# Narrow unread products in TensorE's waits of the first routing round, and four wide ones ahead of its list in place of eight

## The reference

```python
logits = x @ w_gate
flat = logits.flatten()
order = np.argsort(-flat)
for idx in order:
    tok, e = (int(idx) // E, int(idx) % E)
    if assigned[tok] >= 0 or counts[e] >= cap:
        continue
    assigned[tok] = e
    counts[e] += 1
out = np.zeros((N, D), dtype=np.float32)
for e in range(E):
    mask = assigned == e
    h = np.maximum(x[mask] @ w1[e], 0.0)
    out[mask] = h @ w2[e]
```

## Time and profile before

| what | us |
|---|---|
| median of 3 runs | 1098.61 |
| lowest, highest | 1098.16, 1103.46 |
| the profiled execution | 1097.65 |
| its span in the trace | 1095.7 |
| TensorE busy in it | 1056.4 |
| VectorE busy in it | 597.8 |

### The profile page before, as it was taken

The page is one execution under the profiler, slowest core; times in us unless marked ns, Lnnn a source line. Parts: engine busy times, 40 slices in busy tenths (PEclk is TensorE's granted clock), DMA queues, the critical chain, the costliest instruction groups (busy, mean ns, idle before and its releaser), DMA issues. The chain is left out here.

```text
span 1095.7 us, 20355 instructions
## 1 busy us (share of the span) xinstructions
PE 1056.4 (96%) x7565; PEld 903.8 (82%) x7565; DVE 597.8 (55%) x2189; ACT 460.5 (42%) x1172; POOL 422.7 (39%) x472
## 2 busy tenths in 40 slices
PE   9899999999999999999999999948999998999998
PEld 7688888888888888888888888837777786779987
DVE  6754747464747475656556554365675755653110
ACT  5765444444444444444444432203333333234442
POOL 1363222222222222222222224206476647567873
PEclk9999999999999999999999999959999999999999
DMA  6663112121212121212120000014334343324420
GB/s 192 211 206 134 56 56 74 54 70 40 70 55 74 55 73 35 71 55 74 49 70 30 30 11 20 1 38 165 127 143 153 135 156 106 135 97 151 176 106 29
DMA packets 23251, 98.20 MB, mean 90 GB/s; under 512 B 3008, under 2 KB 5056, under 8 KB 20960
## 3 DMA queue, kind: packets, MB, share of 16 engines
q0 software_dynamic: 9824, 58.99, 15.2%
q1 hardware_dynamic: 13328, 37.90, 10.6%
HBM read 84.30 MB, written 12.85 MB: 89 GB/s over the span
## 5 line engine op out<-in xcount | busy, mean ns | idle before, releaser
L427 POOL TENSOR_TENSOR g_low<-g,g_high 128x256 fp32r<-128x256 f32 x192 | 155.1, 808 | 470.8 <-ACT g_high L646 470.7
L536 PE MATMUL up_ps<-x_high,w_high 128*128 128x256 f32 x768 | 227.7, 296 | 0.0
L536 PE MATMUL up_ps<-x_low,w_high 128*128 128x256 f32 x768 | 216.1, 281 | 0.0
L536 PE MATMUL up_ps<-x_high,w_low 128*128 128x256 f32 x768 | 215.1, 280 | 0.0
L814 DVE SCALAR_TENSOR_TENSOR g<-g,up_ps 128x256 f32<-128x256 f32 x192 | 80.4, 419 | 237.0 <-ACT g L639 237.0
L646 ACT ACTIVATE g_high<-g 128x256 fp32r<-128x256 f32 x192 | 80.3, 418 | 209.7 <-PE down_ps L549 140.6
L536 PEld LDWEIGHTS up_ps<-x_high,w_high 128*128 128x128 f32 x768 | 144.5, 188 | 10.7 <-issue 7.7
L549 PE MATMUL down_ps<-w_high,g_high 128*128 128x512 f32 x384 | 152.1, 396 | 0.5 <-POOL g_low L427 0.5
L549 PE MATMUL down_ps<-w_high,g_low 128*128 128x512 f32 x384 | 151.4, 394 | 0.0
L549 PE MATMUL down_ps<-w_low,g_high 128*128 128x512 f32 x384 | 151.2, 394 | 0.0
L536 PEld LDWEIGHTS up_ps<-x_low,w_high 128*128 128x128 f32 x768 | 144.8, 189 | 2.7
(11 more groups left out here) (222 smaller groups left out, 1836.5 us busy)
## 6 DMA issues: line engine op xcount, KB each, us to landing
qk_t<-qk_rows SPq DMA_DIRECT2D x20, 720.0 KB, 4.3
v_w<-v_win SPq DMA_DIRECT2D x40, 232.0 KB
w_raw<-weights SPq DMA_DIRECT2D x16, 512.0 KB, 5.7
x_rest<-x_any POOLq DMA_DIRECT2D x24, 256.0 KB, 3.1
x_rows<-x POOLq DMA_DIRECT2D x12, 512.0 KB, 3.2
w_raw<-gate_rows SPq DMA_DIRECT2D x1, 2048.0 KB, 7.2
qk_t<-qk_rows SPq DMA_DIRECT2D x3, 512.0 KB, 4.4
v_w<-v_win SPq DMA_DIRECT2D x8, 128.0 KB
```

Source lines behind the costliest of these rows:

```text
L427: pool.tensor_tensor(g_low[:, u % 2, :], g[:, u % 2, :], g_high[:, u % 2, :].bitcast(F32), ALU.subtract)\
L536: last = nc.tensor.matmul(up_ps[:, u % 2, 0:GT * P], a[:, f, w], x[:, grp % 2, c, :], start=k == 0, stop=k == 3 * C - 1)
```

## The change

`keep_busy` takes a number of columns, by default 96, half of what it had. The loop over the parts of round 0 is written out, and unread products are put between its parts: 11 narrow ones ahead of the first count, one between a count and its digit, four between a digit and the next count (two after the last digit), three behind the count of the wins, two between the list and its spread. Ahead of the list stand four of 192 columns in place of eight. The 17 behind the spread stay.

```diff
-            def keep_busy(count):
+            def keep_busy(count, columns=T * E // 2):
 
 
                 for _ in range(count):
-                    nc.tensor.matmul(down_ps[:, CT - 1, 0:T * E], ident[:, :], logits[:, :], start=True, stop=True)
-
-            for k in range(SPREAD + 1):
-                route(0, k)
-                if k == SUMS:
-                    keep_busy(8)
-                if k == SPREAD:
-                    keep_busy(17)
+                    nc.tensor.matmul(down_ps[:, CT - 1, 0:columns], ident[:, :], logits[:, 0:columns], start=True, stop=True)
+
+            keep_busy(11)
+            for lv in range(NL):
+                count(0, lv)
+                keep_busy(1)
+                digit(0, lv)
+                keep_busy(4 if lv < NL - 1 else 2)
+            count_wins(0)
+            keep_busy(3)
+            sum_marks(0)
+            keep_busy(4, T * E)
+            list_tokens(0)
+            keep_busy(2)
+            spread_tokens(0)
+            keep_busy(17, T * E)
             for p in range(E):
                 products(p)
```

## The result

The changed kernel is slower by half a percent: 1105.51 us as the median of 20 runs (1102.28 to 1113.76), against 1102.11 us for the kernel before, timed beside it in 20 runs (1097.26 to 1107.52). The ratio is 1.0046, with a 95% interval from 1.0025 to 1.0067: about 5 us more, 3 to 7 by the interval. The profiled execution of the changed kernel is one of the long ones, 1113.73 us with a span of 1111.9, so its end says little. The first routing round is read from it.

The account below looks back on a forecast made before the run. The first routing round was taken as bound by a serial TensorE-VectorE chain at the lower clock, and before the list by the filler itself. Terms -1.6 + 0.4 + 0.5 - 0.4 + 0.1 = -1.0 us; forecast 1097.7, range 1095.3 to 1101.5.

Parts of the forecast that it names:

- The list: Ahead of the token list in round 0: four wide products in place of eight, -1.6 us whatever the clock does.
- The price of a filler: A narrow fp32 pass, taken as bound by its weight load: 0.11 us at the upper clock, 0.21 at the lower.
- The entry: 11 fillers ahead of the first count: nothing at the upper clock, +1.2 at the lower; taken as +0.4 us.
- The levels: Fillers between counts and digits: hidden at the upper clock, 0.5 us each at the lower; one of six assumed, +0.5 us.
- lower level throughout: Rival, also the low rival: lower clock for the whole first routing round, +3.7 us, so 1102.3 us; chance 0.12.
- Marks and spread: Wins' products and counts faster, -0.4 us together; two fillers behind the list delay the spread, +0.1 (+0.6 at the lower clock).
- What it passes on: Behind the tokens' indices: the summed -1.0 us moves gathers and second weights as one; the 17 wide fillers stay hidden.
- The rule on idle gaps: Skill's rule blaming clock drops on long idle gaps; by it the clock-holds rival is expected, 1097.2 us, chance 0.23.
- The later stretches at the lower clock: Rival: a clock fall from 907.6 on, costing 1.6 us, vanishes or another appears: 1096.1 or 1099.3 us; chance 0.08.

Follow-up runs that it names:

- no_entry: The changed kernel without the 11 fillers at the entry; one run, 1104.30 us.
- narrow_48: The changed kernel with narrow fillers of 48 columns in place of 96; one run, 1106.24 us.
- list_as_before: The changed kernel with eight wide fillers ahead of the list again and none behind it; one run, 1105.90 us.

## Why the prediction was wrong

**The list** was right in the step and in the price. -1.6 us from eight fillers to four: the list's start moved by 1.61 us relative to the marks' sums, and the tokens are read 4.18 us behind them (742.80 to 746.98), where the prediction had 4.1. Alone it brought 1.3 at the indices, since with four the clock is still low at the list and its spread.

**The price of a filler** was right for a pass: 0.21 us at the lower level was forecast, (4.98 - 0.4) / 21 = 0.22 measured, and the two runs with 48 columns and with bf16 leave the fp32 weight load as what sets it. By the time that the Trainium skill ("TensorE: Matmul & The Clock Gate", section "LDWEIGHTS (loading the stationary operand)") gives for a load, passes would have been bound by streaming, 0.16 us at the lower level; they are 0.22.

**The entry** is where the prediction failed first. "If it rises after some 3 us here" was taken from eight wide fillers and carried to narrow ones. In the profiled execution the clock did not rise and the entry cost 1.46 us, a little more than the +1.2 that the prediction gives for the lower level. In other executions it rose at 717.8, or had not fallen when the fillers began, so this term does vary between 0 and 1.5.

**The levels** hold the error that decides. One level of six at the lower clock was assumed, for +0.5; in the profiled execution all were at it, for +4.92 from the first count to the wins (+4.51 of it in the six distances between counts). Nothing in the rows carried that choice: the only stretches with narrow work, at 709.60, and with gaps, at 904.20, ended in a fall, and the text itself set a level's streaming beside them and found it thin. The rival "lower level throughout" was given 0.12. It is what the profiles of the changed kernel, of no_entry and of narrow_48 show, and list_as_before, where the clock fell in the first level, comes to nearly the same (wins 21.42 us behind the first count). In nine of the 20 runs the clock was up for some part of the round, and yet even the lowest of the 20, 1102.28 us, lies above the range. The rival's price was also low, 3.1 us for the six levels in place of 4.51: counts are 3.27 us apart, 0.71 more than before and not 0.51. Of that 0.05 is the one filler between count and digit (digit 1.27 us behind the count in place of 1.22; 1.35 in the first level), which was thought to fit by 0.07. The other 0.66 lies between digit and next count, which are 2.00 us apart where the sum for four fillers had 1.80 and the kernel before has 1.34; the passes have the length that was forecast, so the missing 0.2 lies before the first of them and behind the last.

**Marks and spread.** With the clock low the -0.4 was not there but +0.3, and the spread's step cost +0.87 where +0.6 was named for that case.

**What it passes on.** The forecast held that the 17 wide fillers stay hidden. At the lower clock they last 8.51 us and end last, +0.88. So the low rival, at +3.7, measures +7.0 in the profiled execution: +1.46 at the entry, +4.92 in the levels, +0.31 at the marks, -1.61 at the list, +0.87 and +0.21 at the spread, and this +0.88.

**The rule on idle gaps** of the Trainium skill ("TensorE: Matmul & The Clock Gate", section "Why this matters for your kernels") is not enough here. TensorE had no idle time from 713.6 to 740.4 and stayed at the lower level; in the run with the wide entry the clock fell behind two levels with 6.14 busy us of 6.70 and no wait over 0.18 us.

**The range.** The sum itself, -1.0 from 1098.61, gives 1097.6 and not the 1097.7 of the forecast, which changes nothing. The range missed the median, 1105.5 us, for a second reason: the kernel before itself was at 1102.1 us in the same session, and 1098.61 was the median of three. The later stretches at the lower clock were priced at 1.6 us for 3.4, or 0.47 us per us; the line through the 20 runs gives 0.29. But they come as long as 13.7 us, and the forecast allowed for one of 3.4. About 5 us of loss by the ratio is still outside what the forecast's own case allowed.

What stays open: whether the changed kernel itself meets more stretches at the lower clock in the experts than the kernel before, beyond chance. Its 20 runs have a middle of 42 us at the lower level, of which the round alone explains 41 in the profiled execution, and the kernel before met long stretches in one of 20, eight of 19 and three of 23 runs of its three later sets (44 us or more at the lower level). The version with two fillers a level met one in five of five; what brings it on is not shown. Nor do the runs show what makes the clock rise or fall at the entry: it rose under the 11 narrow fillers in one execution and stayed low under them in others.

## What to carry to other kernels

A filler in a gap of the critical chain must fit the gap at the low clock, because that is the clock that this gap had before the filler came; price it by the distance of passes at that level, weight load included, and treat a clock that it may win back as a bonus. Busy is not enough: look for a row in which the very same work, with the same gaps and counts between, raised or held the clock before a term is built on it. And where filler stands directly ahead of work that others wait for, take it away first: that was worth 1.3 us here, the only gain in the round that a timing bears out.

## What the runs showed of the hardware

TensorE busy without a pause can stay at half the clock for long: 21.90 of 21.90 us with narrow fp32 fillers and short counts, and 13.60 of 13.60 us with the expert's own products of 384 columns and counts between them. A pass with 128 columns of fp32 weights takes 0.22 us at the lower level whether 48 or 96 columns follow (22 passes in 4.90 and in 4.98 us), and 0.11 at the upper with 96, (2.67 - 0.28) / 21; a bf16 pass of 128 columns takes (2.50 - 0.2) / 21 = 0.11 us at the lower. The moment at which the clock falls behind the dense layer differed by executions of nearly the same program: at 712.4, 713.1, 714.4, 714.8 and 718.8 us of the span. And the same kernel's time moves by 10 us from run to run, and goes with the stretches at the lower level that it happens to meet.
